# Last chunk's rows for expert 0 placed from the top slot down by 224-column products; ScalarE and VectorE loops written out; split of the attention's pair rows moved

## The reference

```
for e in range(E):
    for k in range(2):
        mask = top2[:, k] == e
        h = np.maximum(x[mask] @ w1[e], 0.0)
        out[mask] += top2_w[mask, k, None] * (h @ w2[e])
```

## Time and profile before

| | us |
|---|---|
| median of three runs | 920.22 |
| the profiled execution | 920.53 |
| its span, first to last instruction | 918.80 |
| attention, to the first product of the feed-forward layer | about 285 |
| feed-forward layer, to the first row turned of the last chunk | 558.7 |
| last chunk's routing, to the first product of expert 0 | 575.95 |

### The profile page before, as it was taken

One profiled execution on the slowest core, in us unless ns is written; L12 is line 12 of the kernel. 1 busy time (PEld: TensorE's weight loads), 2 busy tenths in 40 slices (PEclk: granted clock), 3 DMA queues, 4 the chain that ended last, 5 costly groups with the idle time before them and its releaser, 6 DMA issues.

```text
span 918.8 us, 12569 instructions
## 1 busy us (share of the span) xinstructions
PE 895.6 (97%) x4353; PEld 733.7 (80%) x4355; DVE 524.8 (57%) x953; ACT 427.5 (47%) x701; POOL 142.4 (15%) x147
## 2 busy tenths in 40 slices
PE   6999999999999999999999999999999999999995
PEld 4677777777777888888888888888888888888884
DVE  6787887878866444446444646534445344534453
ACT  4567767677677222343234323333434243433350
POOL 2021221221222000002200240500000000005072
PEclk7999999999999999999999999999999999999999
DMA  5133341432543422414531352626253544527473
GB/s 125 35 86 90 98 123 45 126 95 52 180 147 121 145 101 92 138 47 148 174 126 56 133 179 95 221 95 214 88 177 102 192 143 134 171 91 274 145 247 127
DMA packets 84302, 119.00 MB, mean 130 GB/s; under 512 B 19258, under 2 KB 47930, under 8 KB 84256
## 3 DMA queue, kind: packets, MB, share of 16 engines
q1 hardware_dynamic: 79328, 104.08, 35.2%
q0 software_dynamic: 4928, 14.35, 4.5%
HBM read 89.12 MB, written 29.39 MB: 129 GB/s over the span
## 4 chain that ended last, share of the span: by engine, by line
PE 85%; DVE 7%; ACT 2%; issue 2%; another core or an unknown queue 2%; POOL 1%; DMA 0%; SPq 0%; POOLq 0%; DVEq 0%; ACTq 0%
PE psum L904 10%; PE psum L906 10%; PE psum L905 10%; PE psum L820 10%; PE psum L919 9%; PE psum L921 9%; PE psum L920 9%; PE psum L785 3%; PE psum L805 3%; PE psum L806 3%; DVE neg_max L1444 2%; PE psum L916 1%; PE psum L917 1%; PE psum L1076 1%
## 5 line engine op out<-in xcount | busy, mean ns | idle before, releaser
L820 PE MATMUL psum<-probs,vx 128*128 128x386 f32 x384 | 155.5, 487 | 0.1
L919 PE MATMUL psum<-down_hi,hid_hi 128*128 128x512 f32 x384 | 151.2, 394 | 1.9 <-DVE hid_hi L1767 1.9
L921 PE MATMUL psum<-down_hi,hid_lo 128*128 128x512 f32 x384 | 149.9, 390 | 0.0
L920 PE MATMUL psum<-down_lo,hid_hi 128*128 128x512 f32 x384 | 149.9, 390 | 0.0
L1321 ACT ACTIVATE hid_hi<-psum 128x448 fp32r<-128x448 f32 x64 | 34.8, 545 | 178.3 <-PE psum L906 147.8
L1143 ACT ACTIVATE probs<-psum 128x384 f32<-128x384 f32 x192 | 90.3, 489 | 53.6 <-PE psum L806 51.5
L1767 DVE SCALAR_TENSOR_TENSOR hid_lo<-psum,hid_hi 128x384 fp32r<-128x384 f32 x64 | 35.7, 557 | 122.5 <-ACT hid_hi L1321 115.3
L1444 DVE TENSOR_REDUCE neg_max<-psum 128x1 f32<-128x768 f32 x96 | 91.3, 955 | 24.2 <-PE psum L785 20.5
L1287 ACT ACTIVATE gelu<-psum 128x512 f32<-128x512 f32 x48 | 28.7, 598 | 156.2 <-PE psum L906 146.5
L904 PE MATMUL psum<-sx_hi,up_hi 128*128 128x448 f32 x256 | 93.7, 366 | 1.0 <-issue 1.0
L805 PE MATMUL psum<-qa,ka 102*128 102x384 f32 x192 | 93.3, 486 | 0.5 <-DVEq L1457 0.5
(11 more groups left out here) (209 smaller groups left out, 1544.8 us busy)
## 6 DMA issues: line engine op xcount, KB each, us to landing
raw<-in_moe_w SPq DMA_DIRECT2D x64, 512.0 KB
raw<-in_moe_w_in SPq DMA_DIRECT2D x24, 512.0 KB
raw<-in_moe_w_out SPq DMA_DIRECT2D x24, 512.0 KB
slot_x<-zeros SPq DMA_DIRECT2D x7, 1024.0 KB, 5.5
slot_rows<-slot_x SPq DMA_DIRECT2D x8, 768.0 KB
raw_q<-in_q SPq DMA_DIRECT2D x30, 192.0 KB, 3.3
raw_k<-in_k SPq DMA_DIRECT2D x30, 192.0 KB, 3.7
slot_y<-y_sb SPq DMA_DIRECT2D x7, 768.0 KB, 3.6
```

The lines of the kernel that those rows point to most:

```text
L820: mm(psum[:, 5 + half, 0:WIDE], vx[:, n % 2, c], probs[:, at % SLOTS], start=(c == 0), stop=(c == J - 1)).then_inc(unit_done, 1)
L919: mm(dst, hid_hi[:, held, cols], down_hi[:, slot, f % GP], start=(f == 0), stop=False)
L920: mm(dst, hid_hi[:, held, cols], down_lo[:, slot, f % GP], start=False, stop=False)
L921: return mm(dst, hid_lo[:, held, cols], down_hi[:, slot, f % GP], start=False, stop=(f == pieces - 1))
```

## The change

In four parts: (1) the moves have 224 columns instead of 448 (`WINDOW`) and fill expert 0 from slot 447 down; VectorE masks the slots that are taken (`open_slots`), and the ranks of these rows are turned into slots from the top (`top_ranks`). (2) VectorE's order at the last chunk: all four `turn_lo` before the slots, and weights, rounds and redirect beside piece f = 2 of expert 0. (3) ScalarE's and VectorE's loops over chunks and over experts 0 to 6 are written out. (4) `pair_hi` at units 4 and 5, and GpSimd's second `pair_lo` behind `refine` of the even head.

```
-            return xt_hi[:, j, CT:CT + CAP]
+            return xt_hi[:, j, CT:CT + WINDOW]
...
                     if n % 2 == 0:
                         pair_lo(n - 1, 0)
-                        pair_lo(n - 1, 1)
                 refine(n, 0)
+                if n and n % 2 == 0:
+                    pair_lo(n - 1, 1)
...
-            chain.link(nc.gpsimd.iota(slot_i[:], pattern=[[1, CAP]], base=-FAR, channel_multiplier=0))
+            chain.link(nc.gpsimd.iota(slot_i[:], pattern=[[-1, WINDOW]], base=WINDOW, channel_multiplier=0))
...
-                dst = psum[:, turn_bank(c, True), 0:CAP]
+                dst = psum[:, turn_bank(c, True), CAP - WINDOW:CAP]
...
-                    elif u in (1, 4) and n % 2 == 0:
-                        pair_hi(n - 1, u // 4)
+                    elif u in (4, 5) and n % 2 == 0:
+                        pair_hi(n - 1, u - 4)
...
-            with act.Fori(1, CHUNKS - 1) as t:
+            for t in range(1, CHUNKS - 1):
                 chunk(t, lambda f: route(t - 1, f))
...
-                with act.Fori(0, E - 1) as e:
-                    expert_step(r * E + e, False, r * E + e - skipped)
+                if skipped:
+                    with act.Fori(0, E - 1) as e:
+                        expert_step(r * E + e, False, r * E + e - skipped)
+                else:
+                    for e in range(E - 1):
+                        expert_step(e, False, e)
...
+                open_slots(chain)
                 select(p, at, chain, LAST)
                 first_moves(p, chain, LAST)
-                def turn_half():
-
-                    for c in range(DC // 2):
-                        turn_lo(0, c, True)
-
-                place(p, at, chain, LAST, turn_half)
-                for c in range(DC // 2, DC):
+                rank_rows(p, at, chain, LAST, True)
+                for c in range(DC):
                     turn_lo(0, c, True)
+                give_slots(at, chain)
+
+            def open_slots(chain):
+
+                dve.wait_ge(slot_of_set, 1)
+                chain.link(dv.tensor_scalar(room[:], base[:, 0:1], -1.0, float(CAP), ALU.mult, ALU.add))
+                chain.link(dv.scalar_tensor_tensor(out=slot_open[:], in0=slot_of[:], scalar=room[:], in1=slot_of[:],
+                                                   op0=ALU.is_le, op1=ALU.mult))
...
-                    dv.tensor_scalar(moves(j), slot_of[:], key[:, 1, j:j + 1], None, ALU.is_equal)\
+                    dv.tensor_scalar(moves(j), slot_open[:], key[:, 1, j:j + 1], None, ALU.is_equal)\
                         .then_inc(moves_ready, 1)
+
+            def top_ranks(chain, held):
+
+                full, below, inside, both, moved, taken = (top[:, i] for i in range(6))
+                own_rank = psum[:, held, RANK0:RANK0 + TPC * E].rearrange("p (j e) -> p j e", e=E)[:, :, 0]
+                total = r_rank[:, :, 0]
+                chain.mark(dv.tensor_scalar(below, own_rank, float(WINDOW), None, ALU.is_lt))
+                chain.mark(dv.tensor_scalar(full, total, float(CAP), None, ALU.is_lt))
+                chain.mark(dv.tensor_tensor(both, own_rank, total, ALU.add))
+                chain.mark(dv.tensor_scalar(late[:], psum[:, held, RANK0 + TPC * E:RANK0 + TPC * E + 1], float(WINDOW),
+                                            float(CAP), ALU.is_gt, ALU.mult))
+                chain.pause()
+                chain.mark(dv.tensor_tensor(inside, full, below, ALU.mult))
+                chain.mark(dv.scalar_tensor_tensor(out=moved, in0=full, scalar=float(CAP), in1=total, op0=ALU.mult,
+                                                   op1=ALU.add))
+                chain.pause()
+                chain.link(dv.scalar_tensor_tensor(out=taken, in0=both, scalar=1.0, in1=inside, op0=ALU.add,
+                                                   op1=ALU.mult))
+                chain.link(dv.tensor_tensor(total, moved, taken, ALU.subtract))
...
-            def place(p, at, chain, held, between=None):
+            def place(p, at, chain, held):
+
+                rank_rows(p, at, chain, held, False)
+                give_slots(at, chain)
+                give_weights(p, at, chain)
...
-            with dve.Fori(1, CHUNKS) as t:
+            for t in range(1, CHUNKS):
...
+            def last_weights(f):
+
+                if f != 2:
+                    return
+                give_weights(CHUNKS - 1, bass.ds((CHUNKS - 1) * TPC, TPC), chain)
...
+                else:
+                    for e in range(E - 1):
+                        expert_step(e, False, e, beside=last_weights if e == 0 else None)
```

More of the change, by code:

```diff
@@ L40 @@
 STAGES = 2
+WINDOW = CAP // 2
 LEAD = 1
@@ L230, in clustered_attention_ffn_moe @@
         r_pick = alloc(ffn, "r_pick", [P, 2, TPC, E], F32)
-        slot_i = alloc(ffn, "slot_i", [P, CAP], I32)
-        slot_of = alloc(ffn, "slot_of", [P, CAP], F32)
+        slot_i = alloc(ffn, "slot_i", [P, WINDOW], I32)
+        slot_of = alloc(ffn, "slot_of", [P, WINDOW], F32)
+        slot_open = alloc(ffn, "slot_open", [P, WINDOW], F32)
+        room = alloc(ffn, "room", [P, 1], F32)
+        top = alloc(ffn, "top", [P, 6, TPC], F32)
+        late = alloc(ffn, "late", [P, 1], F32)
         key = alloc(ffn, "key", [P, 2, TPC], F32)
@@ L1591, in route_last @@
                         .then_inc(split_lo, 1)
+                open_slots(chain)
                 select(p, at, chain, LAST)
                 first_moves(p, chain, LAST)
-                def turn_half():
-                    for c in range(DC // 2):
-                        turn_lo(0, c, True)
-                place(p, at, chain, LAST, turn_half)
-                for c in range(DC // 2, DC):
-                    turn_lo(0, c, True)
+                rank_rows(p, at, chain, LAST, True)
+                for c in range(DC):
+                    turn_lo(0, c, True)
+                give_slots(at, chain)
[4 more added lines that the diff above has]
+                                                   op0=ALU.is_le, op1=ALU.mult))
             def first_moves(p, chain, held):
-                chain.link(dv.scalar_tensor_tensor(out=key[:, 0], in0=r_one[:, 0, :, 0], scalar=-float(FAR),
-                                                   in1=base[:, 0:1].broadcast_to((P, TPC)), op0=ALU.mult, op1=ALU.add))
-                dve.wait_ge(slot_of_set, 1)
+                chain.link(dv.tensor_scalar(key[:, 0], r_one[:, 0, :, 0], -float(FAR), float(FAR + 1), ALU.mult, ALU.add))
                 dve.wait_ge(rank_ready, p + 1)
@@ L1652, in select, with rank_rows @@
                 chain.pause()
-            def place(p, at, chain, held, between=None):
+            def place(p, at, chain, held):
+                rank_rows(p, at, chain, held, False)
+                give_slots(at, chain)
+                give_weights(p, at, chain)
+            def rank_rows(p, at, chain, held, from_top):
                 dve.wait_ge(rank_ready, p + 1)
@@ L1659, in place @@
                     base[:].rearrange("p (o e) -> p o e", o=1).broadcast_to((P, TPC, E)), ALU.add))
+                if from_top:
+                    top_ranks(chain, held)
                 for x in range(2):
@@ L1667, in place, with give_slots @@
                 chain.pause()
+            def give_slots(at, chain):
                 slots(at, chain)
@@ L1673, in place, with give_weights @@
                 dve.sem_inc(slots_ready, 1)
-                if between:
-                    between()
+            def give_weights(p, at, chain):
                 dve.wait_ge(gap_exp, p + 1)
@@ L1744, in _, with expert_step @@
             route_last(CHUNKS - 1, chain)
[L1746 to L1757, removed]
+            def last_weights(f):
+                if f != 2:
+                    return
+                give_weights(CHUNKS - 1, bass.ds((CHUNKS - 1) * TPC, TPC), chain)
+                chain.link(dv.tensor_tensor(base[:, 0:1], base[:, 0:1], late[:], ALU.add))
+                chain.link(dv.reduce_max(r_t[:, 0, 0:1], base[:], AX.X))
+                chain.link(dv.tensor_scalar(r_t[:, 1, 0:1], r_t[:, 0, 0:1], float(CAP), None, ALU.is_gt))
+                for x in range(2, ROUNDS):
+                    chain.link(dv.scalar_tensor_tensor(out=r_t[:, 1, 0:1], in0=r_t[:, 0, 0:1], scalar=float(CAP * x),
+                                                       in1=r_t[:, 1, 0:1], op0=ALU.is_gt, op1=ALU.add))
+                dv.tensor_copy(more_rounds[:], r_t[:, 1, 0:1]).then_inc(rounds_ready, 1)
+                for half in range(2):
+                    chain.mark(dv.tensor_scalar(redirect[:, half], slot_all[:, half], float((E - 2 + half) * CAP),
+                                                float(DUMP), ALU.is_ge, ALU.mult))
+                chain.pause()
+                dv.tensor_tensor(slot_got[:], slot_all[:], redirect[:], ALU.max).then_inc(redirected, 1)
             PIECE0 = CHUNKS * (FF // P)
-            def expert_step(n, last, kept, after=None):
+            def expert_step(n, last, kept, after=None, beside=None):
```

(10 more changed lines are left out.)

## The result

The changed kernel takes 917.15 us (median of 12 runs, 913.24 to 920.54) against 920.07 us for the kernel before, measured with it (12 runs, 918.08 to 923.06): ratio 0.9965, 95% interval 0.9952 to 0.9979, so 2.9 us less. Three later measurements on three chips gave the same kernel 0.9959 [0.9945, 0.9974], 0.9938 [0.9924, 0.9951] and 0.9945 [0.9930, 0.9961], which is 4.0, 5.3 and 5.1 us less by the medians. The forecast was 916.0, 4.2 less, with a range from 913.6 to 919.3.

A forecast was written before the change was run, and what follows sets the result against it. PE, busy 97% of the span, was taken to bound the kernel. Moves 3.2 plus attention 1.0 gave 4.2 us less: 920.53 to 916.3 profiled, 916.0 as median; range 913.6 to 919.3.

The forecast's parts named there:

- The moves' products: Last chunk's routing on PE: 32 products at 0.11 us instead of 0.2025, ending at 572.7, 3.2 us earlier.
- rival C: Moves: short fp32r products cost as plain float32, 0.377 us each, 12.1 us for 32; time 924.9; chance 0.05.
- Expert 0's start: After the moves: expert 0 can start at 572.7; nothing waits for top_ranks or turn_lo, 0.1 to 0.3 us to spare.
- What moved behind: Expert 0: slots, weights, rounds and redirect hidden beside products; scatters from 576.5 to about 592; cost 0.
- The attention: Six even heads (2 to 12) last what odd ones do once pair rows move: 0.9 to 1.0 us less.
- The loops: ScalarE's and VectorE's written-out loops: turns hidden behind products; 0 taken, bounds -0.5 and +1.5 us.
- Rival A: Expert 0's late relu signals, scatters 6 us later: no demand met 914.3 (better half), more 917 to 919; chance 0.15.
- Rival D: The change does not act: products keep 0.2 us apart, PE waits elsewhere as long; 919 to 920; chance 0.06.
- Rival B: top_ranks holds PE by 1 us, or pair rows' delay returns elsewhere (all 1.0 us): 917 to 918; chance 0.12.

The follow-up runs named there:

- the kernel before with the wait: Kernel before, plus GpSimd's refine waiting until VectorE has split the next head's rows (low key rows kb): 922.03 us, ratio 1.0008 [0.9997, 1.0019].
- the second repeat: The changed kernel, unchanged, measured again on the chip of the kernel without idle products: 913.08 us, ratio 0.9938 [0.9924, 0.9951].

## Why the prediction was right, and where it was not

**The moves' products: right.** Forecast 3.2 us, measured 2.9 in stages of the same full clock. The distance was 0.112 (0.11 taken), and 32 took 3.71 instead of 3.5: VectorE's matrices come 0.25 us apart (0.22 taken), which paces the first group at 0.25 a pair. They also started 10.62 us into the stage and not the 10.5 taken. The reasoning from both sides, a floor from the earlier trace rows and proportion from the earlier trace rows, held at 160 and 320 columns as well, and rival C (0.377 us) is refuted. The Trainium skill's rule for isolated matmuls (TensorE: Matmul & The Clock Gate, section "Back-to-back issue gap") gives 96, 136 and 189 ns at 224, 320 and 448 columns; measured were 112, 147 and 202.5, so it is short by 11 to 16 ns each time. The 107 ns that its section "LDWEIGHTS (loading the stationary operand)" gives for 128 columns of weights lie near the floor of 109 to 112.

**Expert 0's start: right.** `top_ranks` took 1.07 us (1.2 taken), the `turn_lo` rows keep ahead of PE, which starts expert 0 straight behind the last move. **What moved behind: right.** The slots, weights and rounds are hidden. The scatters start at 579.47 and the last at 595.51, later than the 576.5 and 592 that I took (of the 3.0 us, 1.8 are the low clock's and 0.8 the whole stage's later start), and PE waits nowhere for it.

**The attention: right in the trace.** Six even heads went from 16.57 to 16.61 down to 16.41 to 16.43, together 1.02 us (0.97 over all heads behind the first); 0.9 to 1.0 was said. In timed runs it doesn't stand out: alone 0.9998 [0.9985, 1.0011], taken away 0.9965 against 0.9959. Executions differ by more than 1.0 us.

**The loops: right.** 0 taken, 1.0002 [0.9993, 1.0011] measured.

**Rival A, late signals: not tied to the change.** Beside the scatters PE lost 1.7 us in the profile before and nothing in the one after, which is the rival's better half; but the kernel with the loops alone, whose scatters stand where they stood, lost nothing there either, nor did the kernel before with the wait, which has late signals elsewhere (2.55 us). Late signals occur with the old code and the new, on some chips' profiles and not on others'. **Rival D: refuted** by the stage's rows. **Rival B: refuted in the stage and in the profile after**, where `top_ranks` holds nothing and no head is longer. Its second half, the delay that comes back at another place in the attention, is what other kernels with the moved pair rows show, up to 2.5 us where 1.0 was taken; whether the move has a part in it is open.

**What the prediction missed** is that the trace of one execution holds terms that the next one doesn't. The routing stage's clock, at full speed in the profile of before, fell in the profile after and cost 16.16 - 14.33 = 1.8 us of the 2.9 that the moves win; the start lost another 1.8. The experts, whose late signals I had read as a property of the kernel, then gave 3.3. The changed kernel's four profiles alone span 44.73 to 47.36 us for the start, 14.52 to 16.16 for the routing and 328.84 to 330.47 for the experts. The first measurement's 2.9 us against 4.2 is such a mixture, and the three later measurements' 4.0, 5.3 and 5.1 lie on both sides of it. Whether the low clock is commoner in the changed kernel is open: it was seen in 11 profiles, two of them with the old products, and not in three, two of these with the old products.

## What to carry to other kernels

An fp32r product with 128 columns of weights cost no less at 160 columns than at 224 (0.112 us): narrow a product down to about there, and then stop. Before you price a difference between two profiles, cut both at the same events and ask of each stretch whether the edits can have touched it; here the routing stage showed 2.9 us and the even heads 1.0, while start and experts moved the span by 1.8 and 3.3 us for reasons that no edit is shown to touch. A wait that the profile calls remote, or a stretch at a lower granted clock, can belong to the execution, as both did here, and needs a second profile before it is put down to the code.

## What the hardware showed that I had not expected

- The granted clock can fall to half (1.2 GHz) in a stretch in which PE is never idle: in the profile after it fell 2.6 us into the gate products of 16 columns, with PE busy 16.16 of 16.16 us, and rose after idle products of 512 columns and eight turns. Three of fourteen profiles kept the full clock in this stage. What decides is open.
- Leaving out idle products let the clock stay low 10.2 us instead of 6.8, and products of 224 columns went from 0.112 to 0.21 us; with four of the eight left it was low for 3.4 us and the stage took 14.38, no more than with all eight in three other profiles (3.4 us low; 14.52, 14.62 and 14.74).
- Where VectorE's kb and GpSimd's `refine` start 26 to 30 ns apart VectorE is held in 18 places of 19, where it is 35 to 53 ns GpSimd is, in all 47; the first costs 0.41 us a head.
- ACT's relu rows can start late though PE's products are done, 4.9 us in the place shown, beside runs of GpSimd's indirect DMAs (one each 1.26 us in the place shown, the last of which ended 848.67 - 847.16 = 1.5 us before the late relu). In the second repeat the same runs of DMAs stand there and nothing is late. What delays them was not settled.
